# Turning the softmax weights of blocks 2 to 5 as 32x32 squares through HBM and DVE instead of on TensorE

## The reference

```python
scores_l = scale * q @ k.T                      # masked to |i - j| < 16
scores_s = scale * q @ k_sum.T + np.log(32)     # k_sum: maximum of each 32 keys
a = softmax(concatenate([scores_l_masked, scores_s]))
x = a @ concatenate([v, v_sum])                 # v_sum: mean of each 32 values
...
h = x @ w_in; x = where(h > 0, h, exp(min(h, 0)) - 1) @ w_out
...
out[t] = gate[t] * (max(x[t] @ w1[e], 0) @ w2[e])   # e = argmax of the cosine logits
```

## Time and profile before

| | |
|---|---|
| median of 3 runs | 536.41 us (536.21 to 536.44) |
| profiled execution, first to last instruction | 534.9 us |
| PE busy | 522.5 us (98%), 3858 instructions |
| DVE busy | 311.8 us (58%), 691 instructions |
| ACT busy | 225.5 us (42%), 506 instructions |
| POOL busy | 91.5 us (17%), 221 instructions |
| DMA | 78220 packets, 49.24 MB |
| TensorE's granted clock, mean | 0.996 |

### The profile page before, as it was taken

How to read it: one execution, slowest core, us unless ns; L and a number is a source line. 1 busy time by engine, 2 the same in 40 slices (tenths; PEclk the granted TensorE clock), 3 DMA queues, 4 the chain that set the end, 5 groups by cost and what they waited for, 6 DMA issues and landing times.

```text
span 534.9 us, 11689 instructions
## 1 busy us (share of the span) xinstructions
PE 522.5 (98%) x3858; PEld 450.1 (84%) x3859; DVE 311.8 (58%) x691; ACT 225.5 (42%) x506; POOL 91.5 (17%) x221
## 2 busy tenths in 40 slices
PE   8799999999999999999999999999999999999995
PEld 7688888888888888888888899888788888888883
DVE  3779898557754565457543567768492374222662
ACT  5677764443543343334432545451351352111440
POOL 6413140032210000000000000101312221111221
PEclk9999999999999999999999999999999999999998
DMA  8999220444211112111000900010955155101000
GB/s 210 266 334 315 47 49 12 94 84 98 78 41 25 22 23 63 25 21 54 3 1 1 354 0 2 22 60 10 364 206 198 44 199 188 39 28 36 20 20 25
DMA packets 78220, 49.24 MB, mean 92 GB/s; under 512 B 61014, under 2 KB 66134, under 8 KB 78176
## 3 DMA queue, kind: packets, MB, share of 16 engines
q1 hardware_dynamic: 75776, 42.37, 27.1%
q0 software_dynamic: 2400, 6.30, 3.6%
HBM read 43.40 MB, written 6.82 MB: 94 GB/s over the span
## 4 chain that ended last, share of the span: by engine, by line
PE 95%; ACT 1%; issue 1%; DMA 1%; SPq 0%; DVE 0%; POOLq 0%; DVEq 0%; ACTq 0%
PE bank L1010 25%; PE bank L1054 9%; PE bank L1061 8%; PE bank L1067 8%; PE bank L1219 5%; PE bank L1265 5%; PE bank L1227 5%; PE bank L1273 5%; PE bank L1221 5%; PE bank L1267 5%; PE bank L988 3%; PE bank L970 3%; PE bank L961 2%; PE bank L1257 2%; PE bank L1120 1%; PE bank L1075 1%
## 5 line engine op out<-in xcount | busy, mean ns | idle before, releaser
L1420 ACT ACTIVATE el<-bank 128x512 f32<-128x512 f32 x48 | 28.6, 596 | 112.5 <-PE bank L1010 112.2
L1738 DVE TENSOR_SCALAR el<-el 128x512 f32<-128x512 f32 x48 | 21.1, 440 | 74.7 <-ACT el L1420 74.7
L1010 PE MATMUL bank<-x_hi,w_hi_parts 128*128 128x256 f32 x376 | 61.1, 285 | 0.0
L1010 PE MATMUL bank<-x_hi,w_lo_parts 128*128 128x256 f32 x376 | 60.2, 282 | 0.0
L1010 PE MATMUL bank<-x_lo,w_hi_parts 128*128 128x256 f32 x376 | 60.1, 282 | 0.0
L1010 PEld LDWEIGHTS bank<-x_hi,w_hi_parts 128*128 128x128 f32 x376 | 53.5, 188 | 3.8 <-issue 0.2
L1054 PE MATMUL bank<-w_hi_parts,g_hi 128*128 128x512 f32 x192 | 54.9, 407 | 0.0
L1061 PE MATMUL bank<-w_lo_parts,g_hi 128*128 128x512 f32 x192 | 52.6, 396 | 0.0
L1067 PE MATMUL bank<-w_hi_parts,g_lo 128*128 128x512 f32 x192 | 52.3, 394 | 0.0
L752 POOL COPY kb<-kT 128x96 f32<-128x96 f32 x96 | 26.2, 315 | 148.3 <-PE bank L961 127.9
L1010 PEld LDWEIGHTS bank<-x_lo,w_hi_parts 128*128 128x128 f32 x376 | 51.4, 188 | 0.0
(11 more groups left out here) (288 smaller groups left out, 905.7 us busy)
## 6 DMA issues: line engine op xcount, KB each, us to landing
raw<-in_moe_w SPq DMA_DIRECT2D x8, 2048.0 KB, 7.6
w_raw<-in_moe_w_in SPq DMA_DIRECT2D x8, 512.0 KB, 6.0
w_raw<-in_moe_w_out SPq DMA_DIRECT2D x8, 512.0 KB, 6.6
v_raw<-in_v SPq DMA_DIRECT2D x8, 384.0 KB, 4.0
x_rows<-x SPq DMA_DIRECT2D x6, 512.0 KB, 3.1
vwin<-in_v SPq DMA_DIRECT2D x32, 72.0 KB, 2.1
q_raw<-in_q SPq DMA_DIRECT2D x64, 32.0 KB, 1.9
k_raw<-in_k SPq DMA_DIRECT2D x8, 192.0 KB, 3.2
```

What stands on the lines that cost most here:

```text
L1010: mm = pe.matmul(o, r32(w[:, at:at + P]), r32(x[i % 2][:, c, :]), start=(part == "hh" and c == 0), stop=(part == "lh" and c == DC - 1))
L1420: act.activation(el[n % 2], bank[:, H_BANK[n % 2], :], ACT.Exp).then_inc(e_act, 1)
```

## The change

From unit 8 on the weights are turned as the queries are. The two weight buffers become 128 columns wide for each tile, 8 of them zero, set once by POOL. SP stores a unit's four tiles to a new HBM buffer `p_rows` (256 KB) when they are normalized, and loads them back with four DMAs as squares into `p_squares`; DVE turns the 128x512 in one instruction into `pT` in place p + 2, and the value products wait for that (`p_turned`) instead of ACT's copy. The order of SP's list is rewritten around it. The descriptor space of POOL's DMAs is set to 8192 bytes a partition (16384 if not given).

```diff
+    p_rows = nc.dram_tensor("p_rows", (4, P, P), F32, kind="Internal").ap()
...
-                     + [(p_at(u), 2, u) for u in UNIT_RANGE]
+                     + [(p_at(u), 2, u) for u in UNIT_RANGE if u < 2 * PAIRS]
...
+             "kmaxT": [P, PAIRS, NSUM], "mask": [P, 3, KC], "p_all0": [P, 4, P], "p_all1": [P, 4, P],
+             "p_squares": [P, 4 * P], "pT": [P, 4 * P], "qT0": [P, TB], "qT1": [P, TB], "mean_rows": [P, NSUM]},
...
+            def store_p(u):
+
+                sp.wait_ge(norm_v, u + 1)
+                if u == BY_SQUARES:
+                    sp.wait_ge(p_pads, 1)
+                else:
+                    sp.wait_ge(ld_p, 16 * GROUPS * (u - BY_SQUARES))
+                sp.dma_start(p_rows.rearrange("a p n -> p a n"), p_all[u % 2]).then_inc(st_p, 16)
+
+            def load_p(u):
+
+                sp.wait_ge(st_p, 16 * (u - BY_SQUARES + 1))
+                if u > BY_SQUARES:
+                    sp.wait_ge(p_turned, u - BY_SQUARES)
+                for r in range(GROUPS):
+                    sp.dma_start(p_squares[r * SQ:(r + 1) * SQ, :].rearrange("p (c n) -> p c n", n=SQ),
+                                 p_rows[:, :, r * SQ:(r + 1) * SQ].rearrange("a (t p) n -> p (a t) n", p=SQ)
+                                 ).then_inc(ld_p, 16)
...
-            for u in range(2 * PAIRS, 3 * PAIRS):
+            for u in range(BY_SQUARES, BY_SQUARES + 3):
                 load_q(u)
                 load_windows(u)
...
+            for u in range(BY_SQUARES, UNITS):
+                i, g = divmod(u - BY_SQUARES, PAIRS)
+                if u == BY_SQUARES:
+                    load_q(u + 3)
+                store_p(u)
+                if BY_SQUARES < u < UNITS - 3:
+                    load_q(u + 3)
+                if g == 2:
+                    store_x2(i)
+                load_p(u)
+                if 1 <= u - BY_SQUARES - 2 < PAIRS:
+                    load_v1(u - BY_SQUARES - 2)
+                if 1 <= u - BY_SQUARES - 1 < PAIRS:
+                    load_k1(u - BY_SQUARES - 1)
+                if u < UNITS - 3:
+                    load_windows(u + 3)
...
+            def pads_of_weights():
+                pool.memset(p_all0[:, :, KC:P], 0.0)
+                pool.memset(p_all1[:, :, KC:P], 0.0).then_inc(p_pads, 1)
...
-                pe.wait_ge(pT_ev, u + 1)
+                if u < BY_SQUARES:
+                    pe.wait_ge(pT_ev, u + 1)
+                else:
+                    pe.wait_ge(p_turned, u + 1 - BY_SQUARES)
...
-                for u in STEADY:
+                for u in range(PAIRS, BY_SQUARES):
                     if p_at(u) == place:
                         transpose_p(u)
...
-                for u in STEADY:
+                for u in range(PAIRS, BY_SQUARES):
                     if p_at(u) == place:
                         evacuate_p(u)
...
-                if u >= PAIRS:
+                if u >= BY_SQUARES + 2:
+                    dve.wait_ge(st_p, 16 * (u - 1 - BY_SQUARES))
+                else:
                     dve.wait_ge(p_t, u - 1 if u >= PAIRS + 2 else u - PAIRS + 1)
...
+            def turn_weights(u):
+
+                dve.wait_ge(ld_p, 16 * GROUPS * (u + 1 - BY_SQUARES))
+                dve.wait_ge(o_mm, u)
+                dve.transpose(pT, p_squares).then_inc(p_turned, 1)
...
+                    if p_at(u) + 2 == place:
+                        turn_weights(u)
...
-    nc = bacc.Bacc("TRN2", target_bir_lowering=False, num_devices=1)
+    nc = bacc.Bacc("TRN2", target_bir_lowering=False, num_devices=1, dynamic_dma_scratch_size=8192)
```

More of the change, by code:

```diff
@@ L267, in build @@
         W_HI = W_HI[:, :]
-        (k_raw1, v_raw1, q_raw0, q_raw1, vwin, kT, kb0, kb1, kmaxT, mask, pr0, pr1, pT, qT0, qT1, mean_rows,
+        (k_raw1, v_raw1, q_raw0, q_raw1, vwin, kT, kb0, kb1, kmaxT, mask, p_all0, p_all1, p_squares, pT, qT0, qT1, mean_rows,
          raw, c_sb, iota_m) = zone(
@@ L274, in build @@
              "vwin": [P, PAIRS, WINS, P], "kT": [P, PAIRS, KPAD], "kb0": [P, WINS, KC], "kb1": [P, WINS, KC],
-             "kmaxT": [P, PAIRS, NSUM], "mask": [P, 3, KC], "pr0": [P, 4, KC], "pr1": [P, 4, KC],
-             "pT": [P, 4 * P], "qT0": [P, TB], "qT1": [P, TB], "mean_rows": [P, NSUM]},
+             "kmaxT": [P, PAIRS, NSUM], "mask": [P, 3, KC], "p_all0": [P, 4, P], "p_all1": [P, 4, P],
+             "p_squares": [P, 4 * P], "pT": [P, 4 * P], "qT0": [P, TB], "qT1": [P, TB], "mean_rows": [P, NSUM]},
             {"raw": [P, WSZ], "c_sb": [P, 1536], "iota_m": [P, P]})
@@ L280, in build @@
         q_raw, qT, kb = (q_raw0, q_raw1), (qT0, qT1), (kb0, kb1)
-        pr = (pr0, pr1) + tuple(w_raw[:, at:at + 4 * KC].rearrange("p (a n) -> p a n", n=KC)
+        p_all = (p_all0, p_all1)
+        pr = tuple(a[:, :, 0:KC] for a in p_all) + tuple(w_raw[:, at:at + 4 * KC].rearrange("p (a n) -> p a n", n=KC)
                                 for at in (WALL - 4 * P - 8 * KC, WALL - 4 * P - 4 * KC))
@@ L358, in build @@
             "k_t k_ev k_turned kmx kb_ev q_t q_ev q_turned v_sum m_mm vs_ev")
-        s_mm, mask_h, mask_l, unit_ok, stt, smax, expd, rden_v, rinv_v, norm_v, p_t, pT_ev, o_mm, xh_ev, xl_ev = sems(
-            "s_mm mask_h mask_l unit_ok stt smax expd rden_v rinv_v norm_v p_t pT_ev o_mm xh_ev xl_ev")
+        s_mm, mask_h, mask_l, unit_ok, stt, smax, expd, rden_v, rinv_v, norm_v, p_t, pT_ev, o_mm, xh_ev, xl_ev, p_pads, st_p, ld_p, p_turned = sems(
+            "s_mm mask_h mask_l unit_ok stt smax expd rden_v rinv_v norm_v p_t pT_ev o_mm xh_ev xl_ev p_pads st_p ld_p p_turned")
         emb_a, emb_t, emb_ev, emb_enT, w_hi_a, w_lo_v = sems(
@@ L766, in _ @@
             means_of_rows()
+            pads_of_weights()
             key_columns(6)
```

## The result

The changed kernel takes 530.41 us (median of 4 runs, 530.06 to 530.64), the kernel before 536.31 us on the same chip (536.12 to 536.44): a ratio of 0.9883 (0.9890 by the two medians alone) with a 95% interval of 0.9869 to 0.9897, or 5.5 to 7.0 us less. 530.1 us was forecast.

What follows compares the result with a forecast made beforehand. TensorE's own queue was taken to bound the kernel. Removal gives 6.2 us and additions cost nothing: 534.9 - 6.2 = 528.7 us, plus 1.5 us for the timed median, 530.1 us; range 528.5 to 533.0 us.

Steps and rivals of the forecast that it cites:

- TensorE sets the pace: From 66 to 294 us TensorE is busy 228.00 of 228.00 us; work added elsewhere costs nothing until TensorE waits.
- What the removal gives: Transposes gone in 16 units: 1.50 against 1.12 us, net 0.39 us a unit, 6.2 us; bounds 3.5 and 9.3.
- Rival B: The pause does not reappear at the projection: 9.3 us gained, 527.1 us; chance 8%.
- Why 0.2 us comes back: A pause of 0.16 to 0.20 us, at a semaphore wait behind small products, moves from transposes to projection.
- DVE: One 128x512 transpose a unit, 704 ns, 11.3 us over 16 units, hidden in DVE's idle time.
- SP and DMA: Store and four loads a unit: issuing loads 2.3 us, landing 2.65, store 3.1; the trip is hidden.
- third load of values: Batch 1's value load, issued later behind the weight loads; sums ready 0.6 us before TensorE needs them.
- rival A: Value sums come late, TensorE waits up to 2.4 us at two or three means: 530.5 to 532.5 us; chance 24%.
- Unit 8: Tightest trip, three places instead of five: loads land about 83.2 us, DVE may stall a microsecond, hidden from TensorE.
- the slower rival: Turned weights come late for the value products once a trip exceeds 13 + 3 us: 541.4 us; chance 10%.
- The rest: POOL's pad memsets and halved descriptor space cost nothing; the last stage moves forward as a block, same length.

Runs made afterwards that it cites:

- x1: Changed kernel with four idle transposes put back on TensorE in the same 16 places; 536.44 us, ratio 1.0007 to the kernel before.
- x2: Kernel before without the weight transposes and ACT copies of units 8 to 23, nothing in their place; 530.37 us, ratio 0.9891.
- x3: Changed kernel with each projection's waits moved ahead of the small products in front of it; 530.59 us, ratio 0.9891 to the kernel before.
- y1: Changed kernel with one idle 64x64 product of 64 columns before each of 32 hidden products; 543.17 us, ratio 1.0133 to the kernel before.
- y2: Changed kernel with one idle full 128x128 product of 64 columns before each of 32 hidden products; 536.78 us, ratio 1.0012 to the kernel before.
- y3: Changed kernel with the loads of squares done twice for units 11 to 13; 538.52 us, ratio 1.0035 to the kernel before.
- y4: Changed kernel with squares loaded twice for units 11 to 13 and the value loads put ahead of them; 530.57 us, ratio 0.9895 to the kernel before.
- y8: Changed kernel with the loads of squares done twice for unit 8 alone; 531.90 us, ratio 0.9918 to the kernel before.
- y5: Changed kernel with the loads of squares done three times (three passes) for units 14 to 23; 543.94 us, ratio 1.0153 to the kernel before.
- two passes: Changed kernel with the loads of squares done twice for units 14 to 23; 530.37 us, ratio 0.9899 to the kernel before.
- four passes: Changed kernel with the loads of squares done four times for units 14 to 23; 581.56 us, ratio 1.0843 to the kernel before.

## Why the prediction was right

**TensorE sets the pace.** Right. It is busy all through the edited stretch in both kernels, and x1 and x2 split the change into a removal worth all of the gain and an addition worth nothing.

**What the removal gives.** Right in size: 0.38 us a unit, 16 x 0.38 = 6.1 us, where 0.39 and 6.2 were forecast; the medians give 5.9 and the spans 6.0. The step that carried it was the comparison of one sequence with and without transposes, 1.50 against 1.12 us; taking the 0.58 us of the group would have said 9.3 us. Rival B fell: the third takes 1.12 us in the new places.

**Why 0.2 us comes back.** That one pause moves from the transposes to the projection is right; what causes it is wrong. The prediction had it "paid by whatever waits on a semaphore right behind a run of 16 or 32 small products". x3 took the wait away and the pause stayed; in y1 one small product, with no wait behind it, was enough to bring it up, and y2's full one was not. What the rows before could have told: the scores wait on four semaphores behind 16 small products with no pause, and a projection behind transposes has none. The change between part and full weights fits all of these places. That the number held in spite of the wrong cause is because it was read from a row and not from the mechanism. What inside the array makes the pause is not shown by these runs.

**DVE.** Right: 702 ns against 704 worked out, hidden; no unit waited for it.

**SP and DMA.** The landings were taken a little long: 2.4 us against 2.65 for the loads and 3.1 for the store; issuing four loads took 1.9 against 2.3 us. So the tight places had a little more room than the sum gave them. For the third load of values it gave 0.6 us, and 1.1 was measured: POOL starts 3.7 us after the issue (140.86 to 144.56), as before, so the 0.9 us of backlog in the rings did not show, but the additions took 3.0 us instead of 2.6. The first had 1.4 us, the second 2.2, and rival A didn't come. y3 and y4 show that the place and the mechanism of A were right, and that it hangs on the order in SP's list alone. Unit 8 was placed rightly, 83.6 us for its landing against 83.2 worked out, but partly by luck: the store was issued at 77.38 us and not at 75.7, since the query loads held SP 3.1 us (1.8 before), and quicker issue and shorter landings made up for most of it. DVE came to it 0.9 us later than worked out, at 84.16, behind seven of the small instructions for the embeddings that the sum had put after it. y8 shows that this unit is the first to give way.

**Where the slower rival would begin.** Wrong in its size. The prediction put the point at a trip of more than 13 + 3 us from the unit before, "three times my 5 us". The trip of three passes, 9.4 to 10.4 us of issuing and some 2 us to land, is about 12 us, and it is already slower. Even from "unit u-1 turned" to the squares' landing it is 13.3 us in the last unit of that run (282.74 to 296.00), and 15 us where the query loads stand in between, less than 16 both times. The term missed is that the trips form a loop: the next store waits for the last load, as `p_rows` is single, then come the query loads and then the next loads. The 3 us of spare can be used up once and not in every unit, so the loop has to fit into the time of a unit, 13.2 us (the mean from 84.2 to 281.7 in the changed kernel), and two passes do.

**The rest.** The memsets of the pads, the halved space and the last stage cost nothing; the stretch behind unit 23 is as long as before to 0.1 us.

The Trainium skill, "VectorE: DVE Perf Modes", Rules for kernel authors, leaves a 128x128 transpose on TensorE where PSUM will do as destination. Here a transpose of 128x120 taken off TensorE was worth 0.38 / 4 = 0.1 us, because TensorE was never idle and DVE, SP and the rings had room. The measurement decides for this kernel; with three times the loads in the trip (1.0153 of the kernel before) the rule would have been right.

## What to carry to other kernels

When an engine is busy without a gap, look for two places in its chain that differ in the group to be removed, and price the removal by the difference, since the neighbour's time changes too. Here the transposes could go round through HBM and the vector engine for nothing as long as the whole loop (store, its landing, whatever stands in the queue, the loads) fitted into the time of one unit, about 13 us. Double buffers in HBM and in SBUF should take the waits out of that loop, but no run here tried them. Put loads with a near deadline ahead of those with a far one in an in-order queue: swapping two lines made the difference between y3 and y4, 8 us, with doubled loads.

## What the runs showed of the hardware that was not expected

- A single 64x64 product of 64 columns between full products costs TensorE 0.40 us, a full 128x128 one 0.20 us (y1, y2): going to a part of the array and back costs about 0.2 us, with no wait between the small product and the next full one. Weights of 128x120 do not bring the pause (0.92 us behind them), weights of 128x8 do (3.04 us).
- One wait of 2.33 us on TensorE cost 2.8 us more behind it, since the granted clock was then 0.50 for about 6 us (y3). The length of a wait alone does not decide it: with three passes (y5) the clock stayed at 1.00 behind a wait of 2.67 us (223.42) and fell to 0.50 behind one of 2.16 us (239.09). In y8 a wait of 1.0 us was followed by hidden products at their usual 2.84 us. With four passes the clock was 0.88 on average from 160 to 300 us. The Trainium skill, "TensorE: Matmul & The Clock Gate", Part 1: The HAM clock gate, has the same two levels; which waits bring the lower one is not settled by these runs.
